# The last expert's up product behind the seventh's down product, waits for half matrices, two weight places given sooner, and idle products in the waits of the chain

## The reference

```
gate = 1.0 / (1.0 + np.exp(-(x @ w_gate)))      # x: 2304 x 512, w_gate, w_val: 512 x 1536
x2 = gate * (x @ w_val) @ w_out
logits = x2 @ phi                               # 2304 x 32: 8 experts with 4 slots each
d = softmax(logits, axis=tokens); c = softmax(logits, axis=slots)
slot_input = d.T @ x2                           # 32 x 512
for e in range(8):
    h = np.maximum(slot_input[e] @ w1[e], 0.0)  # w1[e]: 512 x 1024
    slot_out[e] = h @ w2[e]                     # w2[e]: 1024 x 512
out = c @ slot_out                              # 2304 x 512
```

## Time and profile before

| | |
|---|---|
| runs | 593.92, 594.77, 596.26 us |
| profiled execution: its time, its span | 594.65 us, 592.9 us |
| mean granted clock of TensorE in it | 0.975 |
| PE busy, share of the span | 549.3 us, 93% |
| DMA: bytes, queue | 70.97 MB, nearly all on SP's queue |

### The profile page before, as it was taken

The page is one execution under the profiler, slowest core; times in us unless marked ns, Lnnn a source line. Parts: engine busy times, 40 slices in busy tenths (PEclk is TensorE's granted clock), DMA queues, the critical chain, the costliest instruction groups (busy, mean ns, idle before and its releaser), DMA issues.

```text
span 592.9 us, 11279 instructions
## 1 busy us (share of the span) xinstructions
PE 549.3 (93%) x4486; PEld 412.9 (70%) x4486; DVE 224.3 (38%) x500; ACT 200.1 (34%) x514; POOL 101.5 (17%) x171
## 2 busy tenths in 40 slices
PE   6787998999999999999999999999999999968963
PEld 5666777777778778777877878787787777824432
DVE  3696851444625252444235244542212220130103
ACT  4554754334243233152324234233233111230103
POOL 7855022141231202121121202110000000000000
PEclk9697999999999999999999999999999999999988
DMA  8567942121220211111020200102504167589958
GB/s 193 151 139 197 340 119 59 43 72 32 64 71 11 61 23 41 43 42 43 21 63 1 63 20 22 23 21 59 228 1 148 66 237 257 202 310 393 400 190 318
DMA packets 86707, 70.97 MB, mean 120 GB/s; under 512 B 61312, under 2 KB 65920, under 8 KB 86656
## 3 DMA queue, kind: packets, MB, share of 16 engines
q1 hardware_dynamic: 86656, 70.25, 37.8%
HBM read 65.52 MB, written 4.72 MB: 118 GB/s over the span
## 4 chain that ended last, share of the span: by engine, by line
PE 83%; DMA 5%; DVE 4%; issue 2%; ACT 2%; POOL 1%; SPq 1%; POOLq 0%; ACTq 0%; DVEq 0%
PE gateb L940 26%; PE valb L940 25%; PE unitb L948 4%; PE unitb L897 3%; DMA ew_low<-in_moe_w_dram 3%; PE unitb L853 3%; PE unitb L860 2%; PE unitb L962 2%; PE unitb L979 2%; PE unitb L888 2%; PE unitb L868 2%; PE unitb L1023 2%; PE unitb L875 2%; PE unitb L881 1%; PE gateb L1041 1%
## 5 line engine op out<-in xcount | busy, mean ns | idle before, releaser
L940 PE MATMUL gateb<-w_hl,xhl 128*128 128x512 f32 x648 | 163.5, 401 | 0.6 <-ACT xhl L588 0.6
L940 PE MATMUL valb<-w_hl,xhl 128*128 128x512 f32 x648 | 162.2, 399 | 0.0
L940 PEld LDWEIGHTS gateb<-w_hl,xhl 128*128 128x128 f32 x648 | 119.3, 190 | 33.6 <-issue 8.9
L940 PEld LDWEIGHTS valb<-w_hl,xhl 128*128 128x128 f32 x648 | 118.6, 188 | 23.8 <-issue 0.2
L659 ACT ACTIVATE hid<-gateb 128x512 f32<-128x512 f32 x54 | 32.3, 598 | 170.1 <-PE gateb L940 170.1
L779 DVE SCALAR_TENSOR_TENSOR hid<-hid,valb 128x512 f32<-128x512 f32 x54 | 37.1, 688 | 126.6 <-PE valb L940 126.6
L577 POOL TENSOR_TENSOR vd<-v 72x256 f32<-72x256 f32 x16 | 12.1, 756 | 168.8 <-PE unitb L881 166.5
L588 ACT ACTIVATE hT<-unitb 128x512 f32<-128x512 f32 x54 | 32.0, 597 | 21.2 <-PE unitb L948 21.2
L948 PE MATMUL unitb<-ident,hid 128*128 128x128 f32 x216 | 33.3, 278 | 2.5 <-DVE hid L779 1.7
L762 DVE TENSOR_TENSOR xraw<-unitb,outd 128x192 f32<-128x192 f32 x43 | 15.0, 356 | 53.3 <-PE unitb L897 53.1
L948 PEld LDWEIGHTS unitb<-ident,hid 128*128 128x128 f32 x216 | 24.3, 140 | 7.7 <-issue 4.1
(11 more groups left out here) (174 smaller groups left out, 665.7 us busy)
## 6 DMA issues: line engine op xcount, KB each, us to landing
ew_low<-in_moe_w_dram SPq DMA_DIRECT2D x19, 1024.0 KB, 13.6
ew_high<-in_moe_w_dram SPq DMA_DIRECT2D x13, 1024.0 KB, 7.8
qtok<-in_q_dram SPq DMA_DIRECT2D x32, 144.0 KB, 2.8
ktok<-in_k_dram SPq DMA_DIRECT2D x32, 144.0 KB, 3.0
v<-in_v_dram SPq DMA_DIRECT2D x32, 144.0 KB
out_dram<-outs SPq DMA_DIRECT2D x18, 256.0 KB, 3.0
vloc<-in_v_dram SPq DMA_DIRECT2D x32, 112.0 KB
xraw<-in_moe_w_out_dram SPq DMA_DIRECT2D x12, 256.0 KB, 5.8
```

Of the source, the lines that this page charges most:

```text
L940: last = mm(bank[:, :], xhl[:, i % NX, x, kk, :], w_hl[:, c, m, w, kk, :], start=j == 0, stop=j == len(order) - 1)
```

## The change

Five edits. First, the places of t14 to t17 are 20, 18, 17, 19 rather than 17, 18, 19, 20. Place 20 (tiles 14 and 15 of `xhl`) is waited for with the last val product of tile 15, and place 18 (the low part of val's last chunk) with a new semaphore `low_used`. For it the very last val product takes the 4 matmuls with the low part first, of its 12. Second, PE waits for each half of a matrix just before the matmuls that read it; for this the halves of `w2` are cut otherwise (half c now has rows 256j + 128c to 256j + 128c + 127 for j = 0 to 3). Third, up(7) stands behind down(6). Fourth, 22 products whose result nobody reads (`keep_clock`, ident by rep, 128x128, into gateb[0]) stand in PE's waits: 2 behind the last LG, 8 behind the last LS, 1 behind ELT, 4 behind SL, 2 behind the transposes of `acc`, 3 behind the `w_out` product and 2 behind the product that transposes `sin`. Fifth, the size of the attention's buffers is rounded up to 32 bytes each (38,784 rather than 38,616 bytes, which the spare room takes up, so that no place moves).

```diff
+        assert N_TILES - FIRST == LOW and WO_SLOTS * HALF_TILE == FK * DM and GC == 2 * P
+        W_PLACES = 4 * FC
+        W_PLACE = (ATT_BYTES + X_BYTES + SPARE) // (4 * HALF_TILE)
+        X_PLACE = W_PLACE + W_PLACES
+        VAL_LOW, VAL_HIGH = X_PLACE - 1, X_PLACE - 2
+        first_places = [*range(WO_SLOTS, VAL_HIGH), X_PLACE + 1, VAL_LOW, VAL_HIGH, X_PLACE, *range(X_PLACE + 2, SLOTS)]
...
         def place_of_tile(i):
             if i < FIRST:
-                return WO_SLOTS + i
+                return first_places[i]
             return i - FIRST
...
         def load_tile(sp, i):
             e, m, half = i // 4, i // 2 % 2, i % 2
-            rows = (w1, w2)[m].shape[1] // 2
-            src = (w1, w2)[m][e][half * rows:(half + 1) * rows, :].rearrange("(c p) n -> p c n", p=P)
+            if m == 0:
+                src = w1[e][half * (DM // 2):(half + 1) * (DM // 2), :].rearrange("(c p) n -> p c n", p=P)
+            else:
+                src = w2[e].rearrange("(j c p) n -> p c j n", j=UP_GROUPS, p=P)[half]
...
-        def wait_tiles(pe, m, e):
-            for i in (4 * e + 2 * m, 4 * e + 2 * m + 1):
-                pe.wait_ge(tile_in[place_of_tile(i)], 16 * (2 if i >= FIRST and place_of_tile(i) >= WO_SLOTS else 1))
+        def wait_tile(pe, m, e, half):
+            i = 4 * e + 2 * m + half
+            pe.wait_ge(tile_in[place_of_tile(i)], 16 * (2 if i >= FIRST and place_of_tile(i) >= WO_SLOTS else 1))
...
+            if n < W_PLACE:
                 return
+            if n == VAL_LOW:
+                sp.wait_ge(low_used, 1)
                 return
+            if n < X_PLACE:
+                c, m = divmod((n - W_PLACE) // 2, 2)
+                sp.wait_ge((gate_ready, val_ready)[m], ff_n[TILES - 1, c] + 1)
+                return
+            if n < X_PLACE + NX // 2:
+                last_tile = max(i for i in range(TILES - NX, TILES) if i % NX // 2 == n - X_PLACE)
+                sp.wait_ge(val_ready, ff_n[last_tile, FC - 1] + 1)
+                return
...
+        def keep_clock(count):
+            for _ in range(count):
+                mm(gateb[0][:, 0:P], ident[:], rep[:], start=True, stop=True)
...
                 order = ff_parts(not first)
+                lows = 0
+                if (name, arg) == ("val", (TILES - 1, FC - 1)):
+                    order, lows = sorted(order, key=lambda part: (-part[2], part[1])), KT
...
+                    if j == lows - 1:
+                        last.then_inc(low_used, 1)
...
                 if name == "LG":
                     last.then_inc(unit_ready, 1)
+                    if arg == GROUPS_T - 1:
+                        pe.wait_ge(tanh_done, FC * TILES)
+                        keep_clock(2)
...
+                if arg == GROUPS_T - 1:
+                    keep_clock(8)
...
             def up(e):
-                wait_tiles(pe, 0, e)
                 if e >= 2:
                     pe.wait_ge(relu_done, e - 1)
                 for kk in range(KT):
+                    half, c = divmod(kk, KT // 2)
+                    if c == 0:
+                        wait_tile(pe, 0, e, half)
...
-                if e + 1 < NE:
+                if e + 1 < NE - 1:
                     up(e + 1)
-                wait_tiles(pe, 1, e)
                 pe.wait_ge(hT_done, e + 1)
                 for c in range(GC // P):
+                    wait_tile(pe, 1, e, c)
...
                 last.then_inc(w2_used, 1)
+                if e + 1 == NE - 1:
+                    up(e + 1)
```

More of the change, by code:

```diff
@@ L260, in build, with room @@
         HALF_TILE = KT * FE // 2
-        ATT_BYTES = 4 * (2 * NT * 2 * D + 2 * S + 3 * NQ * KW + NQ * P + NQ * 2 * D + 4 * POOL * D + 4 * D
-                         + SD + D - DQ + SD + ND * SD + 2 * ND * 2 * DQ + SD + 3 * NQ + 3 * ND)
+        def room(*sizes):
+            return sum(-(-4 * n // 32) * 32 for n in sizes)
+        ATT_BYTES = room(NT * 2 * D, NT * 2 * D, S, S, 2 * NQ * KW, NQ * KW, NQ * P, NQ * 2 * D, 4 * POOL * D, 4 * D, SD + D - DQ,
+                         SD, ND * SD, 2 * ND * 2 * DQ, SD, NQ, NQ, NQ, ND, ND, ND)
         X_BYTES = 4 * KT * RING
@@ L384, in build @@
         val_ready = sem("val_ready")
+        low_used = sem("low_used")
         tanh_done = sem("tanh_done")
@@ L498, in load_tile, with tile_rows @@
             e, m, half = i // 4, i // 2 % 2, i % 2
-            rows = (w1, w2)[m].shape[1] // 2
-            src = (w1, w2)[m][e][half * rows:(half + 1) * rows, :].rearrange("(c p) n -> p c n", p=P)
+            if m == 0:
+                src = w1[e][half * (DM // 2):(half + 1) * (DM // 2), :].rearrange("(c p) n -> p c n", p=P)
+            else:
+                src = w2[e].rearrange("(j c p) n -> c p j n", j=UP_GROUPS, p=P)[half]
             n = place_of_tile(i)
[L502 to L507, removed]
-        def wait_tiles(pe, m, e):
-            for i in (4 * e + 2 * m, 4 * e + 2 * m + 1):
-                pe.wait_ge(tile_in[place_of_tile(i)], 16 * (2 if i >= FIRST and place_of_tile(i) >= WO_SLOTS else 1))
-        def tile_end(n):
-            return (n + 1) * 4 * HALF_TILE
+            sp.dma_start(slot(n).rearrange("p (c n) -> p c n", n=(w1, w2)[m].shape[2]), src).then_inc(tile_in[n], 16)
+        def tile_rows(m, e, half, c):
+            return slot(place_of_tile(4 * e + 2 * m + half)).rearrange("p (c n) -> p c n", n=(w1, w2)[m].shape[2])[:, c, :]
+        def wait_tile(pe, m, e, half):
+            i = 4 * e + 2 * m + half
+            pe.wait_ge(tile_in[place_of_tile(i)], 16 * (2 if i >= FIRST and place_of_tile(i) >= WO_SLOTS else 1))
         def wait_place(sp, n):
-            end = tile_end(n)
+            end = (n + 1) * 4 * HALF_TILE
             if end <= ATT_BYTES:
@@ L522, in wait_place @@
             sp.wait_ge(x_lo, TILES)
-            end -= ATT_BYTES + X_BYTES + SPARE
-            if end <= 0:
+            if n < W_PLACE:
                 return
[L526 to L533, removed]
-                return
-            if end <= XHL_BYTES + HT_BYTES:
+            if n == VAL_LOW:
+                sp.wait_ge(low_used, 1)
+                return
+            if n < X_PLACE:
[6 more added lines that the diff above has]
+                return
+            if end <= ATT_BYTES + X_BYTES + SPARE + FC * W_BYTES + XHL_BYTES + HT_BYTES:
                 wait_unit(sp, ("LG", GROUPS_T - 1))
@@ L973, in pe_step @@
                 last.then_inc(unit_ready, 1)
+                if arg == GROUPS_T - 1:
+                    keep_clock(1)
             elif name == "SL":
@@ L981, in pe_step @@
                 last.then_inc(unit_ready, 1)
+                if arg == GROUPS_T - 1:
+                    keep_clock(4)
         up_b, hsT_b, y_b, c_b, so_b = banks[0:2], banks[2:4], banks[4], banks[5:7], (banks[7], banks[0])
@@ L1010, in pe_tail @@
             last.then_inc(sin_ready, 1)
+            keep_clock(3)
             pe.wait_ge(sin_done, 1)
@@ L1021, in up @@
                 for kk in range(KT):
+                    half, c = divmod(kk, KT // 2)
+                    if c == 0:
+                        wait_tile(pe, 0, e, half)
                     for j in range(UP_GROUPS):
                         last = mm(up_b[e % 2][j * NS:(j + 1) * NS, 0:GC], sT[:, kk, :],
-                                  tile_rows(0, e, kk)[:, j * GC:(j + 1) * GC], start=kk == 0, stop=kk == KT - 1)
+                                  tile_rows(0, e, half, c)[:, j * GC:(j + 1) * GC], start=kk == 0, stop=kk == KT - 1)
                 last.then_inc(w1_used, 1)
```

4 lines of the change are left out of this document (2 added, 2 removed).

## The result

| | before | changed |
|---|---|---|
| median of the first measurement | 595.14 us (4 runs, 593.92 to 596.26) | 589.17 us (4 runs, 588.38 to 589.74) |
| ratio, 95% interval | | 0.9893, 0.9869 to 0.9917 |
| profiled execution, its span | 594.65, 592.9 us | 588.38, 586.6 us |
| mean granted clock in it | 0.975 | 0.987 |

The kernel is 6.0 us faster, where 3.7 were forecast, and 589.17 lies outside the range of 590.0 to 593.2. The sign and the mechanism held; the size did not.

What follows compares the result with a forecast made beforehand. The prediction took PE's wait for the last expert's w1 halves, and the slow clock after it, as the bound. From 594.65 us it took 3.8, added 0.1 for idle products and 0.12 for the median: 591.0 us, range 590.0 to 593.2.

Steps and rivals of the forecast that it cites:

- The bound: Last expert's first w1 halves: PE waits 3.3 us for bytes, then up(7) takes 3.50 us at half clock, not 1.93.
- The places: Tile stream from t14: earlier issues fill the DMA hole at 519 to 526; stream 2.9 to 3.4 us sooner, no later hole.
- Rival A: Tile stream's end doesn't move, set by something other than the hole: saving 1.6 us, 593.1 us; chance 12%.
- The sum of the tail: From the transposes of expert 6 to ysum: ysum at 571.05 instead of 574.86, 3.8 us saved, less 0.1 for idle products.
- The order: up(7) behind down(6): exposes the relu (0.6 us), takes down(6) from behind the wait (1.8); counted within the 3.8.
- The half waits: Waits for each matrix half: one more PE wait per product, hidden under matmuls of 1.8 us; taken as nothing.
- The idle products: In PE's waits of the last group: 0.22 to 0.27 us each, 0.1 us in all, and no return visible in the trace.
- rival B: Idle products sit on the path: at 0.44 us each they overflow by 3.8 us, giving 594.6 us; chance 10%.
- They return nothing that this trace shows: Idle products in the last group bring no gain: granted clock is 1.00 from 519 to 564 us without them.
- Sum against the profiled execution's own time: Whole kernel: 594.65 - 3.8 + 0.1 = 590.95, plus the median's 0.12, forecast 591.0 us, range 590.0 to 593.2.
- Rival C: New cut of w2 reads slowly and the kernel ends slower; 616.7 us if its tiles take double; chance 3%.

Runs made afterwards that it cites:

- e4: The changed kernel with t14 to t17 at the places and with the waits of before: 594.32 us, ratio 0.9969 to the kernel before.
- e12: The changed kernel with the wait for DVE's copy last ahead of a down product, as before: 590.27 us in its only run, tail 53.42 us.
- e3: The changed kernel without the 22 idle products: 594.03 us, ratio 0.9978 to the kernel before.
- e1: The kernel before with only the fifth edit, buffer sizes rounded to 32 bytes: 595.90 us against 596.09, ratio 0.9998.
- e11: The changed kernel without the 22 idle products, run again for another profile: 593.95 us, ratio 0.9972 to the kernel before.
- e5: The changed kernel with up(7) back ahead of down(6): 591.03 us against 596.20 before, ratio 0.9909, tail 52.47 us.
- e14: The changed kernel with up(7) back ahead of down(6), measured again: 590.54 us against 595.38 before, ratio 0.9920, tail 52.40 us.
- e6: The changed kernel with both half waits of a matrix ahead of its first matmul: 591.59 us against 596.20 before, ratio 0.9927, tail 53.42 us.
- e8: The changed kernel with three times as many idle products, 66: 599.27 us against 596.20 before, ratio 1.0051.
- e2: The changed kernel unaltered, measured a second time: 591.61 us against 596.09 before, ratio 0.9934.
- e7: The kernel before with only the 22 idle products added: 596.53 us against 596.20, ratio 1.0010, tail 59.03 us.
- e13: The changed kernel unaltered, measured a third time: 590.00 us against 595.38 before, ratio 0.9921.

## Why the prediction was wrong, point by point

- **The bound.** Right: PE waited for the last expert's first halves, and paid the clock behind it. With the places of before (e4) the tail gives back 2.2 us.
- **The places.** Right, just past its upper end: issues at 511.3 and 516.6 (forecast 513.4 and 518.5, less the 2.1 us), stream 3.5 us sooner (forecast 2.9 to 3.4), no later hole. Rival A fell with it.
- **The sum of the tail.** Forecast 3.8 less 0.1, measured 4.14. Of the 0.4 missing, 0.3 are three terms of 0.1: both waits for DVE's copy took 0.72, not 0.82, and from down(6) to the transposes of expert 7 it was 4.16, not 4.27. The first two come from the order of two waits that the change swapped without anyone costing it (e12). The last 0.1 is not the price of the idle products, which was paid (up(0) at 18.99 against 18.89 without them, e3): the profile of before had 1.03 us of stop ahead of the transposes of `acc`, where e1, e3 and e11 have 0.86 to 0.88.
- **The order.** The prediction put it among the gains as one sum with the rest. By itself, with the stream sooner, it costs 0.8 to 0.9 us (e5, e14): its own terms, an exposed relu and copy against a wait that is no longer there, would have said so, had each edit been costed with the others in place.
- **The half waits.** Forecast nothing, measured 0.16 us (e6).
- **The idle products.** Price right (0.22 each in e8, 0.1 in all against e3; rival B fell), return wrong. "They return nothing that this trace shows" was true of the trace and taken for the kernel. In e1 and e11 the clock fell in that chain; without them the changed kernel's median is 2.4 us higher (e3 against e2), and e11's profile has a slip of just that size, while e3's has none. In the kernel before they return nothing that the median tells (e7), and e1 shows why: the transfers end last there. So part of their worth exists only beside the new places.
- **The failed step** is the last one: "Sum against the profiled execution's own time", with a range whose lower edge lay only 1.0 us below the forecast. One profile of before stood for all. Its clock stayed up in the last group's chain and came back soon behind the stop, which the profiles of that kernel with one edit each did not do (the first in e1, the second in e7), and the start of the program, the same in both kernels, let the last val product begin anywhere from 515.3 to 520.4 us (after, e3). The profiled pair's 6.3 us are 4.1 of the tail and 2.1 of such a start; the medians of the second and third measurement are 4.5 and 5.4 us apart. By their intervals the gain is 4.9 to 7.8 us in the first measurement, 2.5 to 5.3 in the second and 3.2 to 6.2 in the third: the forecast's 3.7 lies inside the last two and outside the first. The mean tail of before, e1 and e7 is 57.8, which would put the saving of the tail at 4.5 us and not at one profile's 4.1; that is an estimate from three profiles, two of them of kernels with one edit. That the start has no lasting part in it is what e2 and e13 say (last val product at 518.49 and 515.83, around before's 517.46), and e1 excludes the moved buffers. The part of the scatter that is located is a fall of the clock near 122 us, 1.5 us in 11 of 17 profiles; neither profile of the first pair has it, so their 2.1 us are of the other part, but for 0.4. Why a given execution's clock falls or not stays open.
- **Rival C** fell: the landings are 2.72 us apart with the new cut of `w2`, 2.71 before, and the stream runs at 397 GB/s from 524 to 562 where it had 400.

## What to carry to other kernels

Cost each edit of a set with the others in place: here moving the product was right with the old stream and cost 0.8 us with the new one, and a slip of 2.4 us or more that idle products prevent was swallowed where transfers ended last (e1) and went straight to the end once PE did (e11). A chain of short steps with waits between them has no one duration: look at several executions before writing "the clock is 1.00 there", and give a range that holds the executions, not the profile. Before naming the place that makes executions scatter, hold it against all the profiles there are: three of them pointed to the first 50 us here, and seventeen to a place behind. And state first how far two profiles have already come apart ahead of the first place that the change can touch.

## What the runs showed of the hardware

- The same instructions at the same distances had the granted clock at 1.00 in one execution and at 0.50 in another (before and e3 against e1 and e11); ahead of the fall in e1 PE was busy for 1.51 of 3 us. The Trainium skill, TensorE: Matmul & The Clock Gate, section A second HAM failure mode: psum-queue depth-cycling, describes a kernel whose short idles between groups of matmuls let the clock swing; e1 and e11 agree with that in kind, with no idle over 2.1 us.
- A val product near 120 us takes 2.99 to 3.02 us in six profiles and 3.98 to 4.56 in eleven, with the same stop of 1.45 us ahead of it in all seventeen; in e3 the granted clock from 122 to 124 is 0.54.
- With 22 idle products in its waits the chain of the last group kept a clock of 1.00 in 12 of 12 profiles, without them in two of four.
- Of two waits ahead of a matmul the place matters: 0.72 us from the transposes to the next product with the late wait first, 0.82 with it last (after and e12).
- An idle product of 128x128 by 128x128 float32 costs 0.22 us in a row of 24.
